# A fused recurrence and two feed-forward stages on one core: another order for the first group, another split of the weights, two buffers for scores and decayed state

## What is computed

```python
for t in range(S):                      # S = 768, state is 48 x 48 for each head
    cur = einsum('bhd,bhe->bhde', u * k[t], v[t])
    y[t] = einsum('bhd,bhde->bhe', r[t], state + cur)
    state = w[t][..., None] * state + einsum('bhd,bhe->bhde', k[t], v[t])
h = x @ w_in                            # x: 3072 x 384, w_in: 384 x 2048
g = where(h >= 1, h, where(h <= -1, 0, (h + 1) ** 2 / 4))
x2 = g @ w_out
out = (silu(x2 @ w_gate) * (x2 @ w_val)) @ w2_out      # d_ff = 1536
```

## Time and profile before

| | us |
|---|---|
| median of 3 timed executions | 1004.24 |
| their lowest and highest | 1003.71, 1004.32 |
| profiled execution, its own time | 1008.56 |
| span of that execution in the trace | 1006.5 |
| PE / DVE / ACT / POOL busy | 966.8 / 534.7 / 404.1 / 159.4 |
| first feed-forward matmul (L1081) starts at | 37.63 |
| mean granted TensorE clock | 0.991 of full |

### The profile page before, as it was taken

One profiled execution on the slowest core, in us unless ns is written; L12 is line 12 of the kernel. 1 busy time (PEld: TensorE's weight loads), 2 busy tenths in 40 slices (PEclk: granted clock), 3 DMA queues, 4 the chain that ended last, 5 costly groups with the idle time before them and its releaser, 6 DMA issues.

```text
span 1006.5 us, 17391 instructions
## 1 busy us (share of the span) xinstructions
PE 966.8 (96%) x6874; PEld 945.1 (94%) x6874; DVE 534.7 (53%) x905; ACT 404.1 (40%) x849; POOL 159.4 (16%) x151
## 2 busy tenths in 40 slices
PE   4788999999999999999999999999999999999997
PEld 4677999999999999999999999999999999999997
DVE  7684865857668576675444443334333343433332
ACT  4644645445455454553466322222222222222221
POOL 4583430210302102011045400000000000000000
PEclk9988999999999999999999999999999999999999
DMA  8623332121321213210133301010000101010000
GB/s 248 190 71 101 117 94 85 52 85 43 94 80 57 83 44 94 66 43 2 63 105 85 126 1 48 1 48 1 27 20 0 47 0 47 0 47 0 23 1 25
DMA packets 23203, 59.51 MB, mean 59 GB/s; under 512 B 2656, under 2 KB 11616, under 8 KB 23136
## 3 DMA queue, kind: packets, MB, share of 16 engines
q1 hardware_dynamic: 23136, 58.59, 18.8%
HBM read 49.14 MB, written 9.44 MB: 58 GB/s over the span
## 4 chain that ended last, share of the span: by engine, by line
PE 84%; issue 6%; DVE 5%; POOL 3%; ACT 1%; DMA 0%; DVEq 0%; POOLq 0%; ACTq 0%
PE bank L1081 45%; PE bank L1109 31%; PE bank L1132 2%; PE bank L1154 2%; DVE suf L863 2%; PE bank L1149 1%; POOL w1ilo L615 1%; POOL w1olo L615 1%; PE bank L1124 1%; PE bank L1160 1%; PE bank L1141 1%; DVE glo L950 1%; DVE gate L957 1%; POOL r_k_v_by_token L626 1%; DVE k_r_by_channel L885 1%
## 5 line engine op out<-in xcount | busy, mean ns | idle before, releaser
L950 DVE TENSOR_TENSOR glo<-gate,ghi 128x384 fp32r<-128x384 f32 x224 | 139.0, 621 | 118.9 <-ACT ghi L716 118.0
L716 ACT ACTIVATE ghi<-gate 128x384 fp32r<-128x384 f32 x224 | 117.2, 523 | 201.5 <-DVE gate L969 95.4
L967 DVE TENSOR_TENSOR gate<-bank,gate 128x384 f32<-128x384 f32 x96 | 53.5, 558 | 215.0 <-ACT gate L829 215.0
L1081 PE MATMUL bank<-xhi,w2gv_ahi 128*128 128x384 f32 x480 | 161.3, 336 | 0.0
L1081 PE MATMUL bank<-xlo,w2gv_ahi 128*128 128x384 f32 x480 | 161.3, 336 | 0.0
L1081 PE MATMUL bank<-xhi,w2gv_alo 128*128 128x384 f32 x480 | 161.3, 336 | 0.0
L1081 PE MATMUL bank<-xhi,w1ihi 128*128 128x384 f32 x384 | 130.8, 341 | 11.2 <-POOL w1ilo L615 8.7
L1109 PE MATMUL bank<-ghi,w1ohi 128*128 128x384 f32 x384 | 134.5, 350 | 4.8 <-DVE ring L962 4.7
L829 ACT ACTIVATE gate<-bank 128x384 f32<-128x384 f32 x96 | 47.2, 492 | 227.7 <-PE bank L1081 227.7
L1081 PE MATMUL bank<-xhi,w1ilo 128*128 128x384 f32 x384 | 130.2, 339 | 0.0
L1081 PE MATMUL bank<-xlo,w1ihi 128*128 128x384 f32 x384 | 130.2, 339 | 0.0
(11 more groups left out here) (83 smaller groups left out, 1555.7 us busy)
## 6 DMA issues: line engine op xcount, KB each, us to landing
r_k_v_by_token<-in_rkv_token SPq DMA_DIRECT2D x24, 576.0 KB, 5.2
k_r_by_channel<-in_kr_channel SPq DMA_DIRECT2D x24, 448.0 KB, 4.1
w_by_channel<-in_w_channel SPq DMA_DIRECT2D x24, 226.2 KB, 2.9
ring<-in_w_out SPq DMA_DIRECT2D x28, 192.0 KB, 2.6
x_t<-ring SPq DMA_DIRECT2D x8, 576.0 KB, 3.2
x_raw<-x_t SPq DMA_DIRECT2D x8, 576.0 KB, 4.1
out_t<-ring SPq DMA_DIRECT2D x8, 576.0 KB, 3.1
ring<-in_w_in SPq DMA_DIRECT2D x16, 192.0 KB, 2.6
```

Of the source, the lines that this page charges most:

```text
L716: e.activation(ghi[j % 2][:, :], gate[j % 2][:, :], ACT.Copy).then_inc(M["hi", ph], 1)
L950: e.tensor_tensor(glo[j % 2][:, :], gate[j % 2][:, :], ghi[j % 2][:, :].bitcast(F32), ALU.subtract)\
L967: e.tensor_tensor(q, hid[j % 2][:, 0:T], q, ALU.mult).then_inc(M["t", 2], 1)
L1081: m = e.matmul(out, w_of(a, k), x_of(b_, k), start=start and i == 0, stop=stop and i == total - 1)
```

## The change

1. **First group, order.** The 18 fills of group 0 get an order of their own (`FIRST_FILLS`): ST and KT, AT of the next window come before Y. ACT makes its checks of windows 0 and 1 before the first drain, and decays the state before KT's drain. DVE, POOL and ACT follow with orders of their own. Two of the three checks of group 1 move from ahead of slot 0 into slots 0 and 2; ACT has split 9 chunks (it was 7) when slot 0 starts.
2. **Two buffers.** `att` and `sbar` (decayed state) get a twin; window n uses twin n % 2, and a writer waits for the Y of two windows ago, not of the last.
3. **Split of the weights.** Chunks 3, 7, 11, ..., 31 get their `lo` from DVE (`LO_FIRST`), in the slots 0, 1, 3, 4, 6, 8, 9, 10 of group 0; POOL makes the other 24. POOL's products of group 1 move from behind chunks 10, 13, 16 to 12, 18, 24, its values from behind 12, 15, 18 to 16, 21, 28. The sums of group 1 stand in DVE's slots 2, 4, 6 (2, 4, 7 before).
4. **Scalings.** While group 0 runs: slots 0, 2, 7 (they were 1, 2, 4), the scans in 1 and 4 (0 and 1). For later groups: the scaling of window 0 leaves slot 15, all three stand in 0, 1, 4 (15, 0, 2), the sums in 2, 4, 7 (15, 2, 4). The checks move from slots 8, 9, 10 to 9, 10, 12.

```diff
+FIRST_FILLS = [("KT", 0, 0), ("AT", 0, 0), ("AT", 0, 1), ("ST", 0, 0),
+               ("KT", 1, 0), ("AT", 1, 0), ("AT", 1, 1), ("Y", 0, 0),
+               ("KT", 2, 0), ("ST", 1, 0), ("AT", 2, 0), ("AT", 2, 1),
+               ("Y", 1, 0), ("XT", 0, 0), ("Y", 2, 0), ("XT", 1, 0), ("ST", 2, 0), ("XT", 2, 0)]
...
-SCALE_SLOTS = {0: 1, 2: 2}
-DIAG_SLOTS = {2: 1, 4: 2}
+SCALE_SLOTS = {0: 0, 1: 1, 4: 2}
+DIAG_SLOTS = {2: 0, 4: 1, 7: 2}
-CHECK_SLOTS = {8: 0, 9: 1, 10: 2}
+CHECK_SLOTS = {9: 0, 10: 1, 12: 2}
-SCALE_AFTER = {15: 0}
-DIAG_AFTER = {15: 0}
-SCAN_FIRST = {0: 1, 1: 2}
-SCALE_FIRST = {1: 0, 2: 1, 4: 2}
-DIAG_FIRST = {2: 0, 4: 1, 7: 2}
-HI_DONE = {fill: n for fill, n in zip((8, 11, 14, 17), (1, 3, 5, 7))}
-PRODUCTS_AT = {10: 0, 13: 1, 16: 2}
+CHECK_FIRST = {0: 1, 2: 2}
+SCAN_FIRST = {1: 1, 4: 2}
+SCALE_FIRST = {0: 0, 2: 1, 7: 2}
+DIAG_FIRST = {2: 0, 4: 1, 6: 2}
+DVE_LO = 4
+LO_FIRST = {0: 3, 1: 7, 3: 11, 4: 15, 6: 19, 8: 23, 9: 27, 10: 31}
+PRODUCTS_AT = {12: 0, 18: 1, 24: 2}
+VALUES_AT = {16: 0, 21: 1, 28: 2}
...
-        att = [place(f"att{i}", [P, 4, WIN], F32)[0] for i in range(2)]
+        att = [[place(f"att{i}_{n}", [P, 4, WIN], F32)[0] for n in range(2)] for i in range(2)]
-        sbar, _ = place("state_decayed", [PR, NPAIR, 2 * D], F32)
+        sbar = [place(f"state_decayed{i}", [PR, NPAIR, 2 * D], F32)[0] for i in range(2)]
...
+        def wait_lo(wait, c):
+            if (c + 1) % DVE_LO == 0:
+                wait(wlo_d, (c + 1) // DVE_LO)
+            else:
+                wait(wlo, c + 1 - (c + 1) // DVE_LO)
...
                     if c >= RING:
                         wait(whi, c - RING + 1)
-                        wait(wlo, c - RING + 1)
+                        wait_lo(wait, c - RING)
...
@@ block.vector, ahead of the slots
+            drain_at(0)
             scan_window(0, 2)
             scale_window(0, 2)
+            drain_at(1)
+            drain(0, fill_no(0, "ST", 1), 0)
             diag_sum(0, 1)
+            drain(0, fill_no(0, "Y", 0), 0)
+            drain_at(2)
+            drain(0, fill_no(0, "XT", 0), 0)
+            diag_sum(0, 2)
+            drain(0, fill_no(0, "Y", 1), 0)
             sum_w(0)
+            drain(0, fill_no(0, "XT", 1), 0)
+            suffix_scan(1, 0)
+            drain(0, fill_no(0, "Y", 2), 0)
+            drain(0, fill_no(0, "ST", 2), 0)
+            drain(0, fill_no(0, "XT", 2), 0)
...
@@ block.vector, slot
                         diag_sum(1, DIAG_FIRST[j])
-                    if j == 0:
+                    if j in LO_FIRST:
+                        w1_lo(LO_FIRST[j])
+                    if j == 5:
                         sum_w(1)
...
-                    if j in SCALE_AFTER:
-                        scale_window(g + 2, SCALE_AFTER[j])
-                    if j in DIAG_AFTER:
-                        diag_sum(g + 2, DIAG_AFTER[j])
```

More of the change, by code:

```diff
@@ L502, in load_kr @@
                 if g > 0:
-                    wait(fill, (g - 1) * NF + fill_no("Y", w) + 1)
+                    wait(fill, (g - 1) * NF + fill_no(g - 1, "Y", w) + 1)
                 e.dma_start(kr[:, w, :, :, :], kr_d[g, w]).then_inc(ld["kr", w], 16)
@@ L508, in load_tok @@
                 if g > 0:
-                    wait(fill, (g - 1) * NF + fill_no("ST", w) + 1)
+                    wait(fill, (g - 1) * NF + fill_no(g - 1, "ST", w) + 1)
                     wait(y_out, (g - 1) * NW + w + 1)
@@ L617, in w1_lo @@
             def w1_lo(c):
+                if (c + 1) % DVE_LO == 0:
+                    return
                 t = w1i if c % 2 == 0 else w1o
@@ L681, in decay_first @@
             def decay_first(w):
-                e.wait_ge(fill, fill_no("Y", w - 1) + 1)
+                e.wait_ge(scan, OPS_SCAN * w + 1)
+                e.wait_ge(st_dec, OPS_DECAY * w)
                 e.wait_ge(st_out, 2 * w)
@@ L744, in _ @@
             e.activation(checked[:, 0:1], bad[:, 0:1], ACT.Relu).then_inc(tables, 1)
-            for w in range(NW):
-                check_w(0, w)
-                if w == 0:
-                    drain(0, 0, 0)
+            check_w(0, 0)
+            check_w(0, 1)
+            drain(0, fill_no(0, "KT", 0), 0)
+            check_w(0, 2)
+            drain(0, fill_no(0, "ST", 0), 0)
+            decay_first(1)
+            drain(0, fill_no(0, "KT", 1), 0)
             done = [0]
@@ L754, in more_hi @@
                     done[0] += 1
-            for f in range(1, NF):
-                drain(0, f, 0)
-                if FILLS[f][0] == "KT":
-                    decay_first(FILLS[f][1])
-                if f in HI_DONE:
-                    more_hi(HI_DONE[f])
-                if FILLS[f] == ("XT", 1, 0):
-                    check_w(1, 0)
-            for w in range(1, NW):
-                check_w(1, w)
+            drain(0, fill_no(0, "KT", 2), 0)
+            more_hi(2)
+            decay_first(2)
+            more_hi(3)
+            drain(0, fill_no(0, "XT", 0), 0)
+            more_hi(6)
+            check_w(1, 0)
+            drain(0, fill_no(0, "XT", 1), 0)
+            more_hi(7)
+            drain(0, fill_no(0, "XT", 2), 0)
+            more_hi(9)
             knee(0, 0)
@@ L980, in _, with w1_lo, drain_at @@
             e.wait_ge(zero_p, 3)
+            def w1_lo(c):
+                t = w1i if c % 2 == 0 else w1o
+                e.wait_ge(whi, c + 1)
+                e.wait_ge(raw[c % RING], 16 * (c // RING + 1))
+                e.tensor_tensor(t[1][:, c // 2, :], ring[:, c % RING, :], t[0][:, c // 2, :].bitcast(F32),
+                                ALU.subtract).then_inc(wlo_d, 1)
+            def drain_at(w):
+                for n in range(2):
+                    drain(0, fill_no(0, "AT", w, n), 0)
             for w in range(2):
```

111 lines of the change are left out of this document (64 added, 47 removed).

## The result

The changed kernel takes **1007.11 us** (median, 1004.53 to 1009.28), the kernel before beside it 1004.82 (1003.71 to 1007.41). The ratio is **1.0018, with a 95% interval of 1.0009 to 1.0026**: slower by 0.2%, some 2.3 us by the medians. The forecast was 1001.4 and faster. The time lies in the range, on the wrong side, 5.7 us above the forecast and close to the time given with rival 2, the clock (1007.4).

What follows compares the result with a forecast made beforehand. PE, busy 966.8 of 1006.5 us, bounds the kernel, so only its waits and clock can give time. Removed 24.0, added 17.6 and 3.5 for the clock: -2.9, 1005.7, scaled to the median 1001.4; range 989 to 1009.

Steps and rivals of the forecast that it cites:

- rival 2: Slower by the clock: low stretches at waits a to e in group 0, 3.2 us each, three give 1007.4; chance 0.2.
- The clock: PE's clock in group 0: two low stretches removed, -6.4 us; new ones added, 3.5 us, at 3.2 a stretch.
- the copy-outs: Ends of groups: PE's six waits for DVE's copy-out go, -4.7 us.
- a: Group 0, slot 0: ACT's split of chunk 10 waits for its load; tile_out 1 and 2 wait, sum 4.0 us.
- e: Group 0, slots 10 to 12: DVE waits for ACT's split of chunk 31, then scans; XT waits 3.0 us.
- c: Group 0, slot 4: DVE's scan and sum delay the drains of Y and ST; AT of window 1 waits 3.1 us.
- d: Group 0, slot 6: DVE's sum waits for POOL's products behind chunk 24; PE waits 5.3 us, the surest term.
- b: Group 0, slot 2: chunk 14 waits for DVE's lo of chunk 7; tile_out 4 and 3 wait, sum 2.2 us.
- The waits removed: Wait for knee 0 at the third tile_in, -1.0 us; group 0's waits for POOL and the scaling, -10.2 us.
- Rival 4: Slot 4 of later groups grows past 3.1 us, PE waits there 0.8 in each of six groups, 1006.0; chance 0.05.
- Rival 1: New waits mostly covered: a, b, c vanish, d stays 5.3, e 1.5, sum -14.0, 990.3 us; chance 0.2.
- Rival 3: DVE's splits in group 0 wait for POOL at the port: four cost 1.0 more each, 1005.3 us; chance 0.08.

Runs made afterwards that it cites:

- filled gaps: Dead PE transposes put into three gaps of each kernel: changed kernel 1002.71 us, 0.9973 of before; kernel before 1003.32 us, 0.9977.
- this part alone: Kernel before with only the later groups' scalings, sums and checks moved to their new slots: 999.44 us, ratio 0.9935.
- fourth edit: Changed kernel with the suffix scan of group 1 behind the head's last drain on DVE, measured only together with three other edits: 991.05 us, 0.9861 of before.

## Why the prediction was wrong, step by step

- **The clock: this step failed.** The forecast took 6.4 us away for two low stretches and put 3.5 back, −2.9 in sum, and the whole forecast was −2.9. Runs with filled gaps measure the term as far as they took low clock away: it costs before 2.3 us and after 4.5, so +2.2 (give or take 1.8), not −2.9. All other terms of the forecast come to −24.0 + 6.4 + 17.6 = 0.0; measured with filled gaps they are −0.4 by the ratios. So of the 4.7 us between the forecast's −2.9 and the ratio's +1.8 this term makes 5.1, and the others together give back 0.4. That the others fit so well in sum is in part luck: the head brought less than was said, the copy-outs 1.4 us more, and the waits a to e came out 1.1 shorter than walked.
- **Why it was mis-sized, first: the price of a stretch.** A low stretch of 6.8 us was charged with 3.2 (7.0 − 3.7 is rather 3.3), nearly half its length, as if PE set the time all through it. With the transposes some 12 us of low clock fewer gave 4.5 us after, and some 9 fewer gave 2.3 before: 0.37 and 0.25 for each us, not 0.47 (estimates). The rest of it falls in idle time of PE or is paid by waits behind it, as the profiles above show.
- **Second: the profile.** The earlier trace rows were from an execution 4 us above the median, with its low stretches behind its waits of 3.3 and 3.8. In two others the copy-out of group 0 was 3.6 to 4.0 us earlier. The prediction named that distance and carried it along as a factor for the whole sum. It should have asked which terms were in it: a state of the clock that isn't always there can't be taken away in full.
- **Third: the new gaps.** A gap of 3.3 had lowered the clock, and the walk found three of some 3 us and more (c, d, e). I charged one. All three went with low clock in the profile after, the last at 114.2. A fourth stretch, from 33 to 39 in the gap of 4.02 ahead of the first `tile_in` and behind it, had not been looked for; before has one near this place too in each of its profiles (32 to 35, 35 to 42, 34 to 41), and the prediction left it out. And taking 3 us for the length that counts was wrong: low clock also followed the 2.06 of term a.
- **The waits a to e: right.** Walked 4.0, 2.2, 3.1, 5.3, 3.0, sum 17.6. In PE's timeline a is 1.69 + 1.87 = 3.6, b 0.83 + 0.76 = 1.6, c 3.6, e 3.3. For d, 4.42 stand in the row (16.5 in sum), and the edit that takes it away gains 5.9, the low clock behind it included. Each was taken away by the edit that its chain asked for.
- **The waits removed: right as a list, less so as a sum.** POOL's three and the one for `knee` 0 are gone. But of the 1.28 and the 3.30 nothing and 1.05 were there in the second profile of before, where PE had been slow ahead of them. With filled gaps the slots of group 0 last 80.5 before and 86.2 after, +5.7; the forecast without its clock was −1.0 − 10.2 + 17.6 = +6.4.
- **The copy-outs: right, and undersized.** −4.7 was said; from the copy-out of group 0 to the last there are 6.1 us less (878.2 to 872.1), and this part alone gives 6.5. The waits that the profile named held 4.7, the rest it did not name. Rival 4 falls.
- **The head: 1.7 was said**, for a `tile_in` at 35.9. It is at 36.21 and 37.50 after, at 37.63, 37.33 and 35.58 before: about 0, and 1.1 between the two profiles with filled gaps. The spread is too wide to say more, and the clock has a part in it: PE's matmuls reach their full pace at about 28.7 us in the profile of before that the prediction used, and at about 20.5 in the one with 35.58. The walk was right for one link and missed the next. The suffix scan stands ahead of the drain of Y of window 2 on DVE (31.76 to 33.43), and XT waits 4.02:

```profile
31.76 1.54 DVE L906 TENSOR_TENSOR_SCAN suf<-w_by_channel,last_of_segment 112x516 f32<-112x516 f32 x1
33.33 0.18 DVE L909 RECIPROCAL scan_seed<-suf 112x4 f32<-112x4 f32 x1
33.43 0.54 DVE L988 TENSOR_TENSOR x_by_token<-bank,r_k_v_by_token 128x384 f32<-128x384 f32 x1
```

- **The two buffers: misjudged.** They were to remove a wait "that PE's own order would mostly have covered". In the new order one buffer costs 4.0 us. What PE's old order covers, its new order need not; I had looked at the wait in the old one.
- **The rivals.** Rival 2 came true in place: three stretches and more, and the end of group 0 slipped by 8.9 us in the mean of the profiles (119.6 to 128.5), more than the copy-outs gave back. That its time (1007.4) was hit is partly luck, since its 3.2 for a stretch is too much on both sides of its sum. It had been given 0.2 against 0.47, on the argument that in a and b no gap is over 2.6. That says nothing of c, d and e, a gap well under 2.6 proved enough (2.06 in a), and the count that decides it, three stretches, could be made from the walk. Rival 1 falls, since every wait was there. Rival 3, the port, falls in its size: the splits of chunks 19 and 31 on DVE took 0.55 and 0.56, and the one at 72.68, beside POOL, 0.86, so 0.3 and not 1.0. But the instruction behind a split can pay: `lo` 3 took 1.35 at 57.28 beside POOL, 0.8 more than elsewhere, and `tile_out` 3 waited 0.83 for it (58.77, in term b).

What stays open: what the low clock costs in full, since the transposes removed about half of it. The profiles show low stretches of one kernel at different places from one execution to the next, and nothing here tells what decides them. The fourth edit's 2 us in the head are seen in the profile, and the sum of the times is too coarse to show them; that edit wasn't tried alone.

## What to carry to other kernels

If the profiled execution lies outside the spread of the timed ones, profile again before its waits are priced; a term for the clock should be taken from several profiles, or measured by filling the gaps with dead matmuls. When work is moved off a path, walk every queue that it is moved into up to the next thing that PE needs: here the later groups' part alone was worth 0.65%, and the new waits (terms a to e) and their low clock used up all of it. Such waits in series can be taken away one by one, and here the gains added up within what the intervals can tell.
